# Attention weights turned as two half-array transposes, pieces of keys and values turned before them, and the last steps of the attention stage written out

## The reference

```
# q, k, v: (8, 8, 576, 64); pool = 8, so 72 pooled keys for each head
k_p = k.reshape(B, H, Sp, pool, D).mean(axis=3);  v_p likewise
scores = scale * q @ k_p.T ; minus the row's maximum ; exp
attn = attn / (sum + 1e-9)
x = (attn @ v_p), as 4608 tokens x 512

logits = x @ phi                       # 32 slots
d = softmax of logits over the tokens;  slot_input = d.T @ x
slot_out[e] = relu(slot_input[e] @ w1[e]) @ w2[e]      # 8 experts, 4 slots each
c = softmax of logits over the slots;   y = c @ slot_out

h = relu(y @ w_in) ;  g = s * h * h + b ;  out = g @ w_out   # 512 -> 2048 -> 512
```

## Time and profile before

| | us |
|---|---|
| median of 3 runs | 651.08 (651.07 to 653.16) |
| the profiled execution | 652.01 |
| its span, first to last instruction | 650.2 |
| attention stage | 0 to 190 |
| experts and g | 190 to 241 |
| products | 241 to 650 |
| PE busy, of the span | 627.4 |

### The profile page before, as it was taken

How to read it: one execution, slowest core, us unless ns; L and a number is a source line. 1 busy time by engine, 2 the same in 40 slices (tenths; PEclk the granted TensorE clock), 3 DMA queues, 4 the chain that set the end, 5 groups by cost and what they waited for, 6 DMA issues and landing times.

```text
span 650.2 us, 16697 instructions
## 1 busy us (share of the span) xinstructions
PE 627.4 (96%) x6468; PEld 546.5 (84%) x6468; DVE 481.7 (74%) x796; ACT 449.1 (69%) x754; POOL 124.7 (19%) x126
## 2 busy tenths in 40 slices
PE   6799999999999989999999999999999999999996
PEld 6576777776753348889999999999999999999996
DVE  4788676665446648886888878888888887888876
ACT  1588777776521169986777777777777777777772
POOL 3687897622210020003000000000000000000001
PEclk9699999999999989999999999999999999999999
DMA  9968979584379980001000000000000000000001
GB/s 325 322 198 319 338 238 411 175 328 149 130 274 401 417 332 1 1 1 38 30 33 18 34 16 32 16 32 16 32 16 26 22 31 17 16 32 16 33 19 65
DMA packets 26005, 80.50 MB, mean 124 GB/s; under 512 B 6496, under 2 KB 14688, under 8 KB 23392
## 3 DMA queue, kind: packets, MB, share of 16 engines
q1 hardware_dynamic: 25952, 79.76, 33.0%
HBM read 70.32 MB, written 9.44 MB: 123 GB/s over the span
## 4 chain that ended last, share of the span: by engine, by line
PE 88%; DMA 4%; DVE 3%; POOL 2%; issue 2%; ACT 1%; DVEq 0%; ACTq 0%; POOLq 0%
PE bank L1946 16%; PE bank L1957 16%; PE bank L1947 16%; PE bank L1851 5%; PE bank L1698 4%; PE bank L1624 3%; PE bank L1657 2%; PE bank L1685 2%; PE bank L1874 2%; PE bank L1877 2%; PE bank L1881 2%; PE bank L1787 2%; PE bank L1811 2%; DMA kvbuf<-in_v_dram 2%; PE bank L1728 2%
## 5 line engine op out<-in xcount | busy, mean ns | idle before, releaser
L1378 DVE TENSOR_TENSOR lo_sb<-a_sb,hi_sb 128x896 fp32r<-128x896 f32 x128 | 140.0, 1094 | 57.2 <-PE bank L1957 55.6
L1043 ACT ACTIVATE hi_sb<-a_sb 128x896 fp32r<-128x896 f32 x128 | 122.2, 955 | 76.5 <-PE bank L1947 74.7
L1947 PE MATMUL bank<-w_lo,hi_sb 128*128 128x256 f32 x381 | 96.9, 283 | 0.0
L1946 PE MATMUL bank<-w_hi,hi_sb 128*128 128x256 f32 x381 | 96.9, 283 | 0.0
L1028 ACT ACTIVATE a_sb<-r_sb 128x512 f32<-128x512 f32 x144 | 91.1, 632 | 6.4
L1957 PE MATMUL bank<-w_hi,lo_sb 128*128 128x256 f32 x381 | 87.1, 283 | 0.0
L1021 ACT ACTIVATE r_sb<-bank 128x512 f32<-128x512 f32 x144 | 83.7, 581 | 1.2 <-PE bank L1845 0.6
L1947 PEld LDWEIGHTS bank<-w_lo,hi_sb 128*128 128x128 f32 x381 | 73.1, 192 | 0.0
L1946 PEld LDWEIGHTS bank<-w_hi,hi_sb 128*128 128x128 f32 x381 | 73.1, 192 | 0.0
L854 POOL TENSOR_TENSOR pu_sb<-pu_sb,logits 128x256 f32<-128x256 f32 x1 | 0.7, 741 | 334.5 <-DVE x_sb L1436 334.5
L1946 PE MATMUL bank<-t_early,hi_sb 128*128 128x256 f32 x256 | 64.2, 283 | 0.0
(11 more groups left out here) (213 smaller groups left out, 1330.6 us busy)
## 6 DMA issues: line engine op xcount, KB each, us to landing
early_third<-in_moe_w_dram SPq DMA_DIRECT2D x5, 2048.0 KB, 11.8
kvbuf<-in_k_dram SPq DMA_DIRECT2D x12, 768.0 KB, 5.4
kvbuf<-in_v_dram SPq DMA_DIRECT2D x12, 768.0 KB, 6.6
out_dram<-o_sb SPq DMA_DIRECT2D x36, 256.0 KB, 2.3
qbuf<-in_q_dram SPq DMA_DIRECT2D x8, 1024.0 KB, 8.4
early<-in_moe_w_dram SPq DMA_DIRECT2D x4, 2048.0 KB, 10.6
late<-in_moe_w_dram SPq DMA_DIRECT2D x3, 2048.0 KB, 14.8
after_last<-in_moe_w_dram SPq DMA_DIRECT2D x2, 2048.0 KB, 8.7
```

The source lines that it names most:

```text
L1043: act.activation(hi_sb[:, n % 2, :], a_sb[:, n % ARING, P:2 * CH], ACT.Copy).then_inc(hi_ready, 1)
L1378: dve.tensor_tensor(lo_sb[:, n % 2, :], a_sb[:, n % ARING, P:2 * CH], hi_sb[:, n % 2, :].bitcast(F32), ALU.subtract).then_inc(lo_ready, 1)
L1946: pe.matmul(acc, hi, rhs_hi, start=(k == 0 and (at == AT1 or at % 2 == 1)), stop=False, skip_group_check=True)
L1947: last = pe.matmul(acc, hi, rhs_lo, start=False, stop=False, skip_group_check=True)
```

## The change

1. `ex` is turned in halves. Each unit has sixteen transposes of 64 queries x 72 keys against a 64x64 identity in place of eight of 128 x 72. Those of partitions 0 to 63 use the array's upper rows and go to bank 3, those of partitions 64 to 127 use the lower rows and go to bank 4. ACT waits for both, then evicts bank by bank, 72 x 512 each, as before.
2. The pieces of keys and values are turned before the attention weights of the same step, behind the logits. ACT evicts them in the same step, before `aT`, and no longer at the start of the next step.
3. The PE loop ends after step 38. What remains is written out in an order of its own. The exponential of the last batch's `dl` stands one step earlier in ACT's list. L1744 of the last batch begins when the first half of token weights is evicted.
4. `ex`, `aT` and `vn` change places in memory and `ex` is indexed by `(U + 3) % 13`. The load of matrix 9 no longer waits for `l_ready` and `b_ready`.
5. ACT rounds the first rows of w_out after all four partial sums and the first two evictions to `g_st`.

```
+    GAPS = (128, 192, 896, 736)
+    EX_SHIFT = 3
...
+        def ex_slot(U):
+            return (U + EX_SHIFT) % EXR
+        LAST_LOGITS = UNITS + 3
+        def exp_step(g):
+            return group_step(g) + EXP_AT - (g == B - 1)
...
-            sp.wait_ge(l_ready, UNITS)
             sp.wait_ge(ps_ready, B - 2)
-            sp.wait_ge(b_ready, 2 * (B - 1))
             load_matrix(LAST_SLOT + 1)
...
-                for g in groups_at(n, EXP_AT):
+                for g in groups_with(exp_step, n):
...
-                for i, u in pieces_with(value_step, n - 1):
-                    keep_values(i, u)
-                if n > 1:
-                    for i, u in pieces_with(key_step, n - 1):
-                        keep_keys(i, u)
...
+                if n:
+                    for i, u in pieces_with(key_step, n):
+                        keep_keys(i, u)
+                for i, u in pieces_with(value_step, n):
+                    keep_values(i, u)
...
                 U = n - 3
                 if 0 <= U < UNITS:
-                    for g in range(2):
-                        act.wait_ge(aT_ready, 2 * U + g + 1)
-                        act.activation(aT[:, HB * g:HB * (g + 1), :],
-                                       bank[A_B[g]][0:KEYS, :].rearrange("p (a g) -> p a g", a=HB), ACT.Copy).then_inc(aT_kept, 1)
+                    act.wait_ge(aT_ready, 2 * U + 2)
+                    for half, toks in parts():
+                        act.activation(aT[:, :, toks], bank[A_B[half]][0:KEYS, :].rearrange("k (h t) -> k h t", h=H),
+                                       ACT.Copy).then_inc(aT_kept, 1)
...
             keep_part(0)
             keep_part(1)
-            split(FORDER[0])
             keep_g(0)
             keep_g(1)
             keep_part(2)
             keep_part(3)
+            split(FORDER[0])
...
+            for n in range(LAST_LOGITS):
...
+                U = n - 3
+                if 0 <= U < UNITS:
+                    keep_warm(n, 2)
+                    pe.wait_ge(a_ready, U + 1)
+                    if U:
+                        pe.wait_ge(aT_kept, 2 * U)
+                    for h in range(H):
+                        for half, toks in parts():
+                            last = pe.transpose(bank[A_B[half]][0:KEYS, HALF * h:HALF * (h + 1)], ex[toks, ex_slot(U), h, 0:KEYS],
+                                                ident[toks, toks])
+                            if h == H - 1:
+                                last.then_inc(aT_ready, 1)
...
+            keep_warm(STEPS, 1)
+            logits_of(UNITS - 1)
+            keep_warm(STEPS, 2)
+            fold_logits(UNITS - 1)
+            token_weights(B - 2, 0)
+            keep_warm(STEPS, 1)
+            turn_tops(B - 1)
+            token_weights(B - 2, 1)
+            spread_tops(B - 1)
+            keep_warm(STEPS, 1)
+            turn_weights(B - 2)
+            keep_warm(STEPS, 1)
+            token_weights(B - 1, 0)
+            weighted_values(B - 2)
+            token_weights(B - 1, 1)
+            turn_weights(B - 1)
+            keep_warm(STEPS, 2)
+            weighted_values(B - 1)
```

More of the change, by code:

```diff
@@ L1588, in _, with fold_logits @@
                 pe.matmul(bank[A_B[0]][:, 0:P], ident[:, :], ident[:, :], start=True, stop=True)
-            for n in range(STEPS):
+            def fold_logits(U):
+                e = logits_closed(U)
+                pe.wait_ge(fold_ready, 2)
+                pe.wait_ge(l4_kept, e + 1)
+                misc_free("logits", e + 1)
+                for j in range(1 if is_mixed(U) else 2):
+                    for half, toks in parts():
+                        first = P * j + HALF * half
+                        last = pe.matmul(bank[MISC][toks, SLOTS * j:SLOTS * (j + 1)], l4[:, l4_cols(U)][:, first:first + HALF],
+                                         fold[:, 0, :], start=True, stop=True)
+                last.then_inc(lg_ready, 1)
@@ new lines, in turn_tops, with spread_tops @@
+            def turn_tops(g):
+                pe.wait_ge(pm_ready, 2 * g + 2)
+                misc_free("top", g)
+                pe.transpose(bank[MISC][:, 0:P], pm[:, 1:, :].rearrange("p a s -> p (a s)"), ident[:, :]).then_inc(pmT_ready, 1)
+            def spread_tops(g):
+                pe.wait_ge(top_ready, g + 1)
+                misc_free("row", g)
+                pe.matmul(bank[MISC][:, 0:SLOTS], tops[:, 1, g:g + 1].to_broadcast([P, P]), ident[:, 0:SLOTS],
+                          start=True, stop=True).then_inc(row_ready, 1)
@@ new lines, in turn_weights @@
+            def turn_weights(g):
+                pe.wait_ge(b_kept, 2 * g + (1 if g == B - 1 else 2))
+                if g:
+                    pe.wait_ge(ps_kept, g)
+                for h in range(H):
+                    x = h % HB
+                    if g == B - 1 and h == HB:
+                        pe.wait_ge(b_kept, 2 * g + 2)
+                    last = pe.matmul(bank[B_B][0:KEYS, SLOTS * h:SLOTS * (h + 1)], b_sb[:, h // HB, LANES * x:LANES * x + KEYS],
+                                     fold[:, 0, :], start=True, stop=True)
+                last.then_inc(bT_ready, 1)
@@ L1590, in _ @@
+            for n in range(LAST_LOGITS):
                 U = n - 5
                 if 0 <= U < UNITS and closes_logits(U):
-                    e = logits_closed(U)
                     keep_warm(n, 1)
-                    pe.wait_ge(fold_ready, 2)
-                    pe.wait_ge(l4_kept, e + 1)
-                    misc_free("logits", e + 1)
-                    for j in range(1 if is_mixed(U) else 2):
-                        for half, toks in parts():
-                            first = P * j + HALF * half
-                            last = pe.matmul(bank[MISC][toks, SLOTS * j:SLOTS * (j + 1)], l4[:, l4_cols(U)][:, first:first + HALF],
-                                             fold[:, 0, :], start=True, stop=True)
@@ L1736, in _ @@
[L1736 removed]
+                    token_weights(g, half)
                 for g in groups_with(bT_step, n):
                     keep_warm(n, 1)
[L1739 to L1745 removed]
```

169 lines of the change are left out of this document (77 added, 92 removed).

## The result

| | before | changed |
|---|---|---|
| median of 4 runs, us | 651.08 (649.51 to 653.16) | 662.08 (660.83 to 663.23) |
| profiled execution, us | 652.01 | 660.83 |
| its span, us, and mean granted clock | 650.2, 0.990 | 659.0, 0.981 |
| attention stage, start to the experts' first product, us | 190.11 | 197.94 |

The ratio is 1.0157 (95% interval 1.0119 to 1.0195). I had predicted 640.8, with a range up to 647.5. Rows of before are named by their group, as the earlier trace rows. Lines of the changed kernel have moved: L1657 is now L1748 (queries turned), L1698 is L1780 (weights turned), L1624 is L1722 (scores), L1685 is L1628 (logits), L1533, L1556 and L1567 (pieces) are L1540, L1563 and L1574, and ACT's eviction of `qT` is L874 (was L867).

What follows compares the result with a forecast made beforehand. PE was taken to bound the middle of the attention stage. Terms of -5.0, -0.4, -1.0, -1.4 and -2.5 sum to -10.3 us, taking 651.1 to 640.8; the 8-in-10 range was 636.0 to 647.5.

Steps and rivals of the forecast that it cites:

- What bounds the kernel: Whole kernel: PE, busy 627.4 of 650.2 us; in middle attention steps a microsecond off PE comes off the end.
- The halves: Turning the attention weights: sixteen half transposes take about 0.50 us, 0.65 with the change of shape, against 1.00 before.
- Rivals 2 and 3: Halves' loads overlap only in part, about 649 us, chance 0.09; or go one after the other, 654.5, chance 0.07.
- Term 1: Attention steps 12 to 37: halves save 9.9 us, changes of tile shape cost 4.9, together -5.0 us.
- In this trace PE waits for none of them after 56 us: Attention steps: late-pooled keys or values would delay the halves too, but PE showed no such wait; no size given.
- rival 4: Start of the kernel: PE waits more, the low clock lasts some 10 us longer, costing about 4 us; 645, chance 0.06.
- Term 2: Queries' turning in the attention stage: pieces evicted half a step earlier remove PE's wait for `k_sb`, -0.4 us.
- term 3: Start, at half clock: halves and the earlier piece shorten the chain, -1.0 us (-2.0 to 0).
- Term 4: End of the attention stage: earlier folding less later evictions, -1.4 us (-2.2 to 0).
- Term 5: Before the products: evictions run while w_out loads, products begin 3.1 us earlier, POOL's combination gives some back; -2.5 us.

Runs made afterwards that it cites:

- f2_halves_calm: The kernel before with only the half transposes, and seven expert matrices loaded only after the last queries are turned; 673.32 us.
- f3_before_calm: The kernel before with only seven expert matrices postponed until the last queries are turned; 674.94 us.
- e2_order_alone: The kernel before with only the pieces moved ahead of the attention weights, on PE and in ACT's queue; 655.44 us, ratio 1.0064.
- e9_tail_alone: The changed kernel with full transposes, old piece order and old place of the rounding, leaving the stage's new end and tile places; 651.19 us, ratio 1.0007.
- h3_changed_calm: The changed kernel with seven expert matrices postponed until the last queries are turned; 678.54 us.
- f1_more_code: The kernel before with waits on a long-fired semaphore added to PE's transposes, 448 more instructions in the trace; 658.15 us, ratio 1.0096.
- e1_old_order: The changed kernel with the pieces behind the attention weights again, on PE and in ACT's queue; 653.22 us, ratio 1.0022.
- e3_halves_alone: The kernel before with only the half transposes and ACT's one wait for them; 656.37 us, ratio 1.0052.
- g5_pe_order_alone: The kernel before with the pieces moved ahead of the attention weights on PE only, ACT's order as before; 662.07 us.

## Why the prediction was wrong, point by point

- **What bounds the kernel.** PE did, and the halves did come off its work. What I left out is that PE needs its code in time, and that the step of the earlier trace rows is bound by PE only as long as no other engine is put in between. The kernel before already stood 2.3 us for code (1.30 at 86.4, 1.04 at 148.5 us), in lines that I had seen as "issue" and not asked about.
- **The halves** (predicted 0.50 for sixteen, 0.65 with the change of shape). Right, with a time a little under the forecast. Sixteen take 0.57 behind a piece and 0.61 at worst, the change of shape included. Rivals 2 and 3 are out. Of the two rules of the Trainium skill's page TensorE: Matmul & The Clock Gate that stood against each other, Part 3's holds here: loads in different row groups overlapped, at 0.036 us for one half.
- **Term 1, -5.0 (halves -9.9, changes of shape +4.9).** Near in size where the loads are away, wrong in what it was part of. In f2_halves_calm against f3_before_calm, a step is shorter by 0.17 and 0.23 us in two stretches with pieces (1.56 and 2.06 us over nine steps) and by 0.32 behind them (1.61 over five): -5.8 over 26 units. Single steps gain 0.24 to 0.30, but in others PE comes to the queries before ACT has evicted the last piece, and waits 0.52 instead of 0.20. Beside the loads this gain is lost again to code and clock: the kernel with the halves alone is 4.4 us slower.
- **"In this trace PE waits for none of them after 56 us": the step that failed.** The sentence is true of the kernel before and was carried over to the new order, as if the piece had no other wait. I asked whether keys and values would be pooled in time, and never named the other wait of the piece, `qT_kept`. The piece is written into the bank of the queries, so ACT must have evicted them (0.60, and 0.14 of hand-over). I knew bank 0 as shared, but only thought of the queries that wait for the piece. Before, the weights' 1.00 us and the logits' 0.57 lay between; now the logits alone do, and in steps where ACT first has `vphi`, `dl` and `ex` to do the wait is 0.9. The waits for `qT` went from 0.8 to 9.2 us. Alone the order costs 3.4 us (e2_order_alone), where my sum had nothing but the early eviction's -0.4.
- **Code, a term that was not in the sum.** I counted the sixteen halves by their time on PE and left the 288 more pairs of instructions at nothing. Beside the loads the stands for code went from 1.3 to 7.0 us between units 9 and 30, with up to 3.4 us of low clock behind them, and the halves, forecast at a gain, lost 3.3 to 4.4 us in the old order and 7.8 in the new one.
- **Clock, rival 4** (0.06, +4 us at the start). It did fall, in the middle of the stage and behind stands, at up to 3.4 us of price in the first profile and 6.8 in the second. What I looked at, PE's work at the start, was not what moved. The rule of Part 4 of that page of the Trainium skill, that transposes do not count as PE-busy in the same way, did not matter here: f2_halves_calm ran 58 us with halves in every step at 1.00.
- **Term 2, -0.4, and term 3, -1.0.** 0.7 us was gained to unit 9; the pieces' waits for `qT` began there already.
- **Term 4, -1.4.** 1.0 us from unit 35 to the experts in the profiled executions, 0.4 in the median of e9_tail_alone. The mechanism was right, the size a little over.
- **Term 5, -2.5.** The products began 3.5 us earlier against the experts' start (I had 3.1), 1.0 was left at the third unit, and the clock took up to 1.7. I had allowed 1.1 for POOL's combination; it was 2.5, and the clock came on top. Alone the rounding gave 1.1 us in the median.
- **The sum.** The four parts alone have +3.4, +4.4, -1.1 and -0.4, which is +6.3; together they have +11.0 in the first measurement and +8.6 in the second. The 2 to 5 us more come when halves and order are in one step. h3_changed_calm ties them to the loads, not to the program's waits.

What stays open: why code comes late more often when halves and order are together (no kernel with the order alone stands), what of a stand's cost goes on through the clock in a mean run, and where a median run of f1_more_code loses its time; the traces have one execution for each kernel, but for the changed one.

## What to carry to other kernels

Before a tight loop gets more instructions for less work, count them: here each also had to come in as code over the same DMA engines as the loads, and 448 that do nothing cost about 6 us. The sign is PE idle on "issue" inside a group, with a packet of the instruction queue landing 1.2 to 1.6 us before it goes on; where loads are thin, as in the last eight units here, the same edit pays. And before a step is moved, list every semaphore that it waits for and the bank it writes, not only its input: what used to stand between it and the last reader of that bank was its cover.

## What the runs showed of the hardware

- PE ran dry of code at records 193 over a multiple of 256, all 30 times, and went on 1.2 to 1.6 us after the 16 KB packet had landed. 448 instructions of 51 ns each that do nothing cost 5.7 to 6.5 us with the loads and 2.3 with most of these gone (the last from four runs each).
- Stands of PE between 34 and 185 us of 1.44, 1.48, 1.61, 1.67, 1.68, 2.53, 2.55 and 4.18 us each went with a clock of 1.2 GHz for 3.4 to 20.5 us. PE was fully busy under it in seven of them; in e1_old_order the clock fell at 138.7 us, inside the stand of 4.18. After stands of 1.30, 1.12, 1.11, 1.11, 1.07, 1.04 and 1.03 us it stayed at 2.4 GHz. The cause of the stand was code in six of the eight, POOL in one (1.44) and another wait in one (1.61). In e3_halves_alone it also fell at 164.4 us, behind a stand of 0.75, so this is no sharp rule.
- Sixteen transposes on 64*72 tiles, alternating between the array's row halves, took 0.57 us behind a full-array group (the changed kernel); eight on 128*72 took 0.87 in the same place (g5_pe_order_alone).
